# Attention's own term as scaled copies on ScalarE, and the state's decay folded into the key table and VectorE's state sums

## The reference

```python
def _attn_ref(r, k, v, w, u):            # r, k, v: (4, 8, 768, 48); w, u: (8, 48)
    state = np.zeros((B, H, D, D), dtype=np.float32)
    for t in range(S):
        kt, vt, rt = (k[:, :, t], v[:, :, t], r[:, :, t])
        cur = np.einsum('bhd,bhe->bhde', u[None] * kt, vt)
        y[:, :, t] = np.einsum('bhd,bhde->bhe', rt, state + cur)
        state = w[None, :, :, None] * state + np.einsum('bhd,bhe->bhde', kt, vt)
...
    x = attn_out.transpose(0, 2, 1, 3).reshape(B * S, H * D)      # 3072 x 384
    x = _moe_ref(x=x, **moe_kwargs)      # 8 experts, 384 tokens each, 384 -> 1024 -> 384
    return _moe2_ref(x=x, **moe2_kwargs) # 384 -> 2048 -> 384, relu squared
```

## Time and profile before

| what | us |
|---|---|
| median of 3 runs (878.37 to 878.81) | 878.4 |
| the profiled execution | 878.33 |
| its span on the core | 876.6 |
| start of the tables and first loads | 0 to 16.3 |
| attention, 24 units | 16.3 to about 168 |
| routing of the first expert | about 168 to 213 |
| experts and dense layer | 213 to 876.6 |

### The profile page before, as it was taken

One profiled execution on the slowest core, in us unless ns is written; L12 is line 12 of the kernel. 1 busy time (PEld: TensorE's weight loads), 2 busy tenths in 40 slices (PEclk: granted clock), 3 DMA queues, 4 the chain that ended last, 5 costly groups with the idle time before them and its releaser, 6 DMA issues.

```text
span 876.6 us, 18438 instructions
## 1 busy us (share of the span) xinstructions
PE 811.8 (93%) x6695; PEld 777.4 (89%) x6695; DVE 551.1 (63%) x1159; ACT 290.0 (33%) x581; POOL 328.7 (37%) x312
## 2 busy tenths in 40 slices
PE   5999999624999999999999999999999999999995
PEld 4888888623899999999999999999999999999995
DVE  7999999675777458546845692678358633931210
ACT  1233332103135315422542253235314533542332
POOL 6777677203026303520541063126303520531232
PEclk9999999855999999999999999999999999999998
DMA  8776776013023001200310040022002200400000
GB/s 228 213 220 232 214 250 209 29 51 121 2 73 100 26 2 72 99 27 0 120 50 27 8 162 0 27 72 99 9 18 72 99 27 1 172 1 28 1 1 27
DMA packets 22143, 69.86 MB, mean 80 GB/s; under 512 B 3552, under 2 KB 6752, under 8 KB 22112
## 3 DMA queue, kind: packets, MB, share of 16 engines
q1 hardware_dynamic: 19040, 59.99, 21.2%
q0 software_dynamic: 3072, 9.44, 3.1%
HBM read 59.98 MB, written 9.44 MB: 79 GB/s over the span
## 4 chain that ended last, share of the span: by engine, by line
PE 77%; DVE 11%; issue 5%; POOL 5%; ACT 1%; DMA 0%; DVEq 0%; POOLq 0%
PE bank L1196 16%; PE bank L1197 15%; PE bank L1198 15%; PE bank L1250 8%; PE bank L1252 8%; PE bank L1251 8%; PE bank L1143 3%; DVE ks L638 2%; PE bank L1059 2%; DVE am L645 1%; DVE rs L639 1%; POOL rku L401 1%; DVE hot L802 1%; POOL kn L385 1%; POOL rk L396 1%
## 5 line engine op out<-in xcount | busy, mean ns | idle before, releaser
L469 POOL TENSOR_TENSOR h_lo<-sq,h_hi 128x384 fp32r<-128x384 f32 x128 | 152.9, 1198 | 398.2 <-DVE sq L966 398.1
L966 DVE SCALAR_TENSOR_TENSOR sq<-bank,relu 128x384 f32<-128x384 f32 x128 | 71.0, 555 | 133.6 <-ACT relu L565 133.3
L1250 PE MATMUL bank<-m_hi,h_hi 128*128 128x384 f32 x384 | 132.0, 344 | 0.0
L1196 PE MATMUL bank<-x_hi,m_hi 128*128 128x384 f32 x384 | 130.6, 340 | 0.3
L1252 PE MATMUL bank<-m_hi,h_lo 128*128 128x384 f32 x384 | 129.8, 338 | 0.0
L1251 PE MATMUL bank<-m_lo,h_hi 128*128 128x384 f32 x384 | 129.5, 337 | 0.0
L1197 PE MATMUL bank<-x_lo,m_hi 128*128 128x384 f32 x384 | 129.2, 336 | 0.0
L1198 PE MATMUL bank<-x_hi,m_lo 128*128 128x384 f32 x384 | 129.1, 336 | 0.0
L565 ACT ACTIVATE relu<-bank 128x384 f32<-128x384 f32 x128 | 63.0, 492 | 194.5 <-PE bank L1198 192.3
L559 ACT ACTIVATE h_hi<-bank 128x384 fp32r<-128x384 f32 x64 | 31.5, 492 | 192.1 <-PE bank L1198 192.0
L958 DVE SCALAR_TENSOR_TENSOR h_lo<-bank,h_hi 128x384 fp32r<-128x384 f32 x64 | 35.4, 554 | 72.0 <-ACT h_hi L559 72.0
(11 more groups left out here) (172 smaller groups left out, 1572.4 us busy)
## 6 DMA issues: line engine op xcount, KB each, us to landing
w_raw<-we_in SPq DMA_DIRECT2D x48, 512.0 KB, 4.9
nn<-nn_in SPq DMA_DIRECT2D x24, 576.0 KB, 4.1
tt<-tt_in SPq DMA_DIRECT2D x48, 192.0 KB, 4.9
m_raw<-m_in SPq DMA_DIRECT2D x12, 512.0 KB, 5.7
x_rows<-yrow SPq DMA_DIRECT2D x24, 192.0 KB, 1.9
xg<-x_rows,perm_next POOLq DMA_INDIRECT x24, 4.4
out<-xg,perm_now POOLq DMA_INDIRECT x24, 2.6
u_row<-u_in SPq DMA_DIRECT2D x1, 192.0 KB, 6.0
```

The source lines that it names most:

```text
L469: pool.tensor_tensor(h_lo[g % 3][:, :], sq[g % 2][:, :], h_hi[g % 3][:, :].bitcast(f32), ALU.subtract).then_inc(lo2_ready, 1)
L966: dve.scalar_tensor_tensor(out=sq[g % 2][:, :], in0=h_ps[g % 3][:, 0:CAP], scalar=0.0, in1=relu[:, :], op0=ALU.max, op1=ALU.mult).then_inc ...
L1196: pe.matmul(out, hi_w, hi_x, start=first, stop=False)
L1250: pe.matmul(acc_ps[t][:, 0:DM], h_hi[r][:, s], m2_hi[:, c:c + DM], start=first, stop=False)
```

## The change

- The own term leaves GpSimd. ScalarE makes it as 8 copies (one for each head, 128x48) with a scale that it reads for each partition. They stand at the head of ScalarE's part of a unit, ahead of the copy of the turned output.
- The state's decay leaves ScalarE: the 4 scaled copies and the tile `zt` are gone. VectorE instead runs 4 SCALAR_TENSOR_TENSOR, state = state·w_chunk + increment, in place. They wait for the increment and for the part of the output that reads the state.
- For that to be right the increment has to carry the decay of the chunk: the key table that is transposed is no longer `kpow` but `kpow`·`w_chunk`, one more VectorE operation at the start (112x512), written into `rs[1]`, which is free then. The transposes wait for it.
- TensorE's state_update waits for the new state sum where it waited for `zt`.

```diff
--- before.py
+++ after.py
@@ -50,8 +50,8 @@
 STEPS = [T * T, T, 1]
 FAR = 9999.0
 CLOSED = 1.0e38
-N_TABLE_KPOW = 13
-N_TABLE = 17
+N_TABLE_KPOW = 16
+N_TABLE = 18
 POOL_TILES = 1
 
 COUNTS_AT = G1 + 1
@@ -136,7 +136,6 @@
         own = [sb(f"own{j}", [P, H], f32, att) for j in range(2)]
         ownv = [sb(f"ownv{j}", [P, DM], f32, att) for j in range(2)]
         am = [sb(f"am{j}", [P, 2, 512], f32, att) for j in range(2)]
-        zt = sb("zt", [HD, PAIRS, D], f32, att)
         state = [sb(f"state{b}", [HD, PAIRS * D + P - D], f32, att) for b in range(B)]
         yrow = [sb(f"yrow{b}", [P, DM], f32, att) for b in range(B)]
         yT = sb("yT", [P, DM], f32, att)
@@ -224,7 +223,7 @@
         nn_in = [sem(f"nn_in{b}") for b in range(B)]
         inter_done = sem("inter_done")
         m2_in = [sem(f"m2_in{j}") for j in range(2)]
-        scores_ready, masked, update_ready, z_ready = sem("scores_ready"), sem("masked"), sem("update_ready"), sem("z_ready")
+        scores_ready, masked, update_ready = sem("scores_ready"), sem("masked"), sem("update_ready")
         scaled, own_ready, y_sum, y_ready = sem("scaled"), sem("own_ready"), sem("y_sum"), sem("y_ready")
         rk_ready, rku_ready, ownv_ready = sem("rk_ready"), sem("rku_ready"), sem("ownv_ready")
         kn_ready, state_ready = sem("kn_ready"), sem("state_ready")
@@ -400,20 +399,8 @@
                     pool.wait_ge(own_ready, n - 1)
                 pool.tensor_tensor(rku[j][:, :], rk[:, :], u_row[:, :], ALU.mult).then_inc(rku_ready, 1)
 
-            def own_values(i, b):
-
-                n, j = 4 * i + b, b % 2
-                pool.wait_ge(own_ready, n + 1)
-                if not (isinstance(n, int) and n < 2):
-
-                    pool.wait_ge(y_ready, n - 1)
-                pool.tensor_tensor(ownv[j][:, :].rearrange("p (h d) -> p h d", h=H),
-                                   nn[b][:, 0, :].rearrange("p (h d) -> p h d", h=H),
-                                   own[j][:, :].unsqueeze(2).broadcast_to([P, H, D]), ALU.mult).then_inc(ownv_ready, 1)
-
             def units(i, last):
                 for b in range(B):
-                    own_values(i, b)
                     if last and b == B - 1:
                         continue
                     if last:
@@ -512,16 +499,18 @@
 
             def units(i, last):
                 for b in range(B):
-                    n = 4 * i + b
+                    n, j = 4 * i + b, b % 2
+
+                    act.wait_ge(own_ready, n + 1)
+                    if not (isinstance(n, int) and n < 2):
+
+                        act.wait_ge(y_ready, n - 1)
+                    for h in range(H):
+                        cols = slice(h * D, (h + 1) * D)
+                        done = act.activation(ownv[j][:, cols], nn[b][:, 0, cols], ACT.Copy, scale=own[j][:, h:h + 1])
+                    done.then_inc(ownv_ready, 1)
                     if not is_first(n):
                         turned_y(n - 1)
-                    if not last:
-
-                        act.wait_ge(z_ready, n + 1)
-                        act.wait_ge(inter_done, n + 1)
-                        for p in range(PAIRS):
-                            done = act.activation(state[b][:, p * D:(p + 1) * D], zt[:, p, :], ACT.Copy, scale=w_chunk[:, p:p + 1])
-                        done.then_inc(state_ready, 1)
                     if not is_first(n):
                         gated(n - 1)
                     if b % 2 and not (last and b == B - 1):
@@ -626,6 +615,8 @@
             tab(dve.reciprocal(w_first[:, :], powr[:, :, 0:1].rearrange("p q o -> p (q o)")))
             tabbed()
             tab(dve.tensor_tensor(w_chunk[:, :], w_first[:, :], powr[:, :, P:P + 1].rearrange("p q o -> p (q o)"), ALU.mult))
+            tabbed()
+            tab(dve.tensor_tensor(rs[1][:, :, :], kpow[:, :, :], w_chunk[:, :].unsqueeze(2).broadcast_to([HD, PAIRS, P]), ALU.mult))
             dve.wait_ge(kt_ready, 1)
             for a in range(2):
                 tab(dve.tensor_copy(kpow_n[:, :].rearrange("p (q a d) -> p q a d", q=PAIRS, a=2)[:, :, a, :],
@@ -659,10 +650,13 @@
             def state_sum(i, b):
 
                 n = 4 * i + b
-                dve.wait_ge(state_ready, n + B)
                 dve.wait_ge(update_ready, n + 1)
-                dve.tensor_tensor(zt[:, :, :], state[b][:, 0:PAIRS * D].rearrange("p (q f) -> p q f", q=PAIRS),
-                                  u_ps[0:HD, 0:PAIRS * D].rearrange("p (q f) -> p q f", q=PAIRS), ALU.add).then_inc(z_ready, 1)
+                dve.wait_ge(inter_done, n + 1)
+                for p in range(PAIRS):
+                    c = slice(p * D, (p + 1) * D)
+                    done = dve.scalar_tensor_tensor(out=state[b][:, c], in0=state[b][:, c], scalar=w_chunk[:, p:p + 1],
+                                                    in1=u_ps[0:HD, c], op0=ALU.mult, op1=ALU.add)
+                done.then_inc(state_ready, 1)
 
             def m2_low(i, b):
 
@@ -1039,7 +1033,7 @@
             fill(25, 1)
             pe.wait_ge(table, N_TABLE_KPOW)
             for p in range(PAIRS):
-                last = pe.transpose(tr_ps[:, p * HD:(p + 1) * HD], kpow[:, p, :], ident[0:HD, 0:HD])
+                last = pe.transpose(tr_ps[:, p * HD:(p + 1) * HD], rs[1][:, p, :], ident[0:HD, 0:HD])
             last.then_inc(kt_ready, 1)
 
             def front(i, b):
@@ -1071,7 +1065,7 @@
                 pe.wait_ge(kn_ready, n + 1)
                 if not is_first(n):
 
-                    pe.wait_ge(z_ready, n)
+                    pe.wait_ge(state_ready, n + B)
                 for p in range(PAIRS):
                     for a in range(2):
                         c = slice((2 * p + a) * D, (2 * p + a + 1) * D)
```

## The result

The changed kernel takes 871.7 us (median of 4 runs, 870.98 to 872.39) where the kernel before takes 878.38: a ratio of 0.9923, 95% interval 0.991 to 0.9936. It is 6.7 us faster (0.8%); 870.0 was forecast, with a range of 867.8 to 874.8. The profiled execution is the slowest of the four, 872.39, with a span of 870.7 (before: 878.33 and 876.6). Six more runs later gave 871.21 in the median.

The account below looks back on a forecast made before the run. A VectorE ring of 6.34 us, partly waiting for GpSimd's reads, was taken as the bound, then TensorE at 5.86. 878.3 less 9.3 and 0.1, plus 0.9, gave 869.8, stated as 870.0; range 867.8 to 874.8.

Parts of the forecast that it names:

- the floor: TensorE's row in a unit: 5.36 us to state_update plus 0.50 to the next warm-up, 5.86; TensorE becomes the bound.
- The ring before: Unit before the change: warm-up and scores 1.75 us, mask 1.20, `ks` 1.39, `rs` 1.40, `yrow` 0.60, together 6.34.
- "slower" rival: Attention units: late GpSimd, and VectorE's work outgrows its 0.49 us slack by 0.35 a unit; 886 us, chance 0.07.
- The lock: VectorE with two SBUF inputs and GpSimd reading SBUF exclude each other for the whole instruction; a rule to weigh.
- The state sums: Four VectorE instructions replacing `zt` (0.34 us): 0.6 taken, 0.84 without overlap; covered, ending before the mask.
- ScalarE: Eight copies replacing four in a unit take 1.9 us; cost nothing until a copy takes over 0.4.
- The start: Transposes wait for `w_chunk` and a 112x512 product, until 12.87 us; all behind comes 0.9 us later.
- The first units: `kn` of unit 1 may fall into its `rs`, TensorE's stand before unit 2 may shrink; 0 taken, bounds -1.2 and +1.0.
- Behind the attention: Around the routing, into the first expert's matmuls: TensorE's clock may return at another time; 1.5 us either way.
- The sum: Whole kernel: 878.3 - 9.3 - 0.1 + 0.9 = 869.8 us, given as 870.0.
- The lock does move to `m_lo`: Rival in the units: `m_lo` waits for `kn`, perhaps `rk`; period about 6.1 us, half the gain, 874.5; chance 0.13.
- No gain: Rival: `kn` starts at 1.9 us, GpSimd still meets `ks` and `rs`, period stays 6.35; 879.2 us, chance 0.07.

Follow-up runs that it names:

- late GpSimd run: The changed kernel with a useless product on GpSimd where the own term stood, in all but the last four units: 879.88 us, ratio 1.0017.
- own term alone: The kernel before with only the own term moved to 8 copies on ScalarE, state and key table as they were: 870.08 us, ratio 0.9906.
- state half alone: The changed kernel with the own term back on GpSimd, so only the state in one step is left: 876.22 us, ratio 0.9974.
- second profile: Profiled execution of the unaltered changed kernel from its six later runs: 871.29 us.
- first profile: Profiled execution of the changed kernel from its first four runs: 872.39 us, span 870.7.
- both ends mended: Own term alone moved, plus GpSimd waiting for `yrow` in the last four units and the last own term on GpSimd: median 870.48 us, profiled 868.73.

## Why the prediction was right

**What bounds the kernel, and the floor.** Right for the changed kernel. TensorE no longer waits for `yrow`; its floor was put at 5.36 + 0.50 = 5.86, and the 18 intervals are 5.86 us each. `ks` was forecast held by `rku` until 3.7 us and `rs` ended at 4.9; they were 3.73 and 4.88. The late GpSimd run shows that the place of GpSimd's products decided, and the own term alone shows that no other part of the change was needed.

**The ring before.** Wrong in part. The prediction laid it through warm-up, scores and mask, and its terms do add up to 6.34, but `ks` had a fixed end, that of `rk` and 0.54, and not a fixed length. The path that set the pace ran over GpSimd, as the table above shows. The forecast didn't suffer by it, since the new period was worked out from TensorE's own row, and the remedy, GpSimd's products out of the way, is the same for both rings. But that reading is why the state half alone was expected at 879 to 880, and not at 876.22, and why the "slower" rival had 886.

**The lock.** The Trainium skill, "SBUF — State Buffer", section "Who interferes with whom", has the one issued first win. The traces agree at four places: `m_lo` ends 0.54 behind the end of `kn` (35.17 and 35.71), `ks` 0.55 behind that of `rku`, `rk` is 1.45 long with `m_lo` in between, and with the own term back on GpSimd the order of own term and `m_lo` turned round when `m_lo` was issued 0.4 us later. The state sums are not held: 0.79 with `kn` beside them, 0.77 in the other runs. The prediction used it only as a rule to weigh, and hadn't drawn from it that a longer step in front can help.

**The state sums.** 0.77 to 0.79 for four; I took 0.6 and gave 0.84 as the end. Covered, as said. **ScalarE.** 1.9 for eight copies was forecast, 1.91 to 1.93 measured; inside the loop nothing waits for them, as said.

**The start.** 0.9 forecast, 0.95 measured. **The first units.** Taken at 0 with bounds of -1.2 and +1.0. In the second profile it was -0.22. In the first it was +1.37, outside the bounds: `kn` falling into `rs` was foreseen; that the clock could fall behind the idle time was not, and where it fell it cost 1.5 us. **Behind the attention.** 1.5 us either way was allowed; 0.24 came.

**Terms that were missing.** The last interval with state work, 6.20 in the place of 5.86: I counted 19 equal intervals, but the last one is next to a unit without `kn`, where GpSimd runs on at once. And the tail, 0.47 us: the eight copies cost nothing in a unit of 5.86, but at the end nothing is left to cover them, and `yT` waits. Together 0.8. The run with both ends mended takes both away in its trace.

**The sum.** 869.8 with 9.3 + 0.1 gained and 0.9 lost. Taking the first profile's rows: 18 x 0.487 = 8.77, 0.15 into unit 21 and 0.05 behind it gained; 0.95 at the start, 1.37 in the first units, 0.47 in the tail and 0.24 in the experts lost; net 5.9, from 876.6 to 870.7. The forecast missed the median by 1.7. Of the 2.6 between 869.8 and the profiled 872.39, the first units are 1.37, the tail 0.47, the interval into unit 21 0.34, and the experts 0.24; nothing of it lies in the regular intervals. That the median came so near is partly luck: it lies between two pairs of runs, at 871.0 and 872.4, and how many fall into which isn't in the prediction.

**The rivals.** The lock does move to `m_lo`, which takes 0.95, but it waits for `kn` alone and ends as the mask starts, so it costs nothing; the further hold by `rk` that this rival feared didn't come. No gain and slower didn't come, since `kn` starts 0.23 behind the warm-up; the first is what the late GpSimd run makes. There 0.02 us a unit is left of the gain (6.32 against 6.348).

## What to carry to other kernels

When two engines share a lock, look at what stands at the head of the other engine's row and when it is released: moving that one step, even to an engine where it costs more instructions, can take every later step out of the way. When a step is held by a lock, its end is fixed by the other engine, so follow the chain through that engine before calling the steps in front of it part of the ring. Once another engine is the bound, look again at what was put on it when it was idle; here the warm-up matmuls had come to cost 7.4 us (870.08 against 862.72), though the first units needed some for the clock. And count the first and the last turns of a loop apart, since what is covered inside isn't covered there.

## What the runs showed of the hardware that I had not expected

TensorE's clock was seen to fall behind one idle stretch of 1.5 us early in the program, and not in every execution of the same program: `back` took 3.57 us mostly at 0.50, and 2.05 at 1.00. Ahead of unit 1's scores the stretch was 1.46 us long in four profiles (the changed kernel twice, the own term alone, both ends mended), and the clock fell in one of them. It was 1.68 and 1.99 us long with 2 and with no warm-up matmuls, and the clock fell in both. It was 0.66 us or less in the other six profiles, the kernel before among them, and the clock stayed at 1.00. In the loop it stayed at 1.00 with no warm-up matmuls at all, TensorE being busy for 96.67 of 98 us.

A held instruction ends at a fixed distance behind the one that holds it. `ks` (112x512, 0.68 when free) ended 0.54 to 0.56 us behind `rk`, and `rs` the same behind `rku`, in every unit read of the kernel before and of the two runs above with GpSimd late or the state half alone.
